# A mixture-of-experts kernel on one core: VectorE's order around the final routing, and who makes the first expert's last low parts

## The reference, cut to what matters

```python
logits = einsum('bsd,de->bse', x, w_gate)
local_gate = sigmoid(x @ w_local)
for s in range(S):
    fresh_e = argmax(logits[b, s])
    e = fresh_e if s == 0 or local_gate[b, s] < 0.5 else prev_e
    prev_e = e
    p = softmax(logits[b, s])
    h = maximum(x[b, s] @ w1[e], 0)
    out[b, s] = p[e] * (h @ w2[e])
```

## Time and profile before

| | |
|---|---|
| median of 3 runs (lowest, highest) | 622.44 us (621.17, 623.4) |
| the profiled execution, its own time | 623.0 us |
| its span, first to last instruction | 621.2 us |
| instructions | 14687 |
| TensorE busy | 607.2 us (98%) |
| VectorE busy | 412.6 us (66%) |
| ScalarE busy | 321.5 us (52%) |
| GpSimd busy | 172.5 us (28%) |
| chain that ended last, by engine | TensorE 90%, VectorE 6%, issue 2%, ScalarE 1%, GpSimd 1% |

### The profile page before, as it was taken

One profiled execution on the slowest core, in us unless ns is written; L12 is line 12 of the kernel. 1 busy time (PEld: TensorE's weight loads), 2 busy tenths in 40 slices (PEclk: granted clock), 3 DMA queues, 4 the chain that ended last, 5 costly groups with the idle time before them and its releaser, 6 DMA issues.

```text
span 621.2 us, 14687 instructions
## 1 busy us (share of the span) xinstructions
PE 607.2 (98%) x4483; PEld 504.5 (81%) x4484; DVE 412.6 (66%) x1164; ACT 321.5 (52%) x698; POOL 172.5 (28%) x241
## 2 busy tenths in 40 slices
PE   7989999999999999999999999999999999999996
PEld 6878888888888888889979878788788888888885
DVE  4767779845888797786979958957735335463541
ACT  5767779768516614632544844637526225362531
POOL 4545545600000000000000231285632521544141
PEclk9999999999999999999999999999999999999999
DMA  8987786002120010000004751886933512754000
GB/s 307 377 272 249 268 288 212 18 2 85 57 80 0 1 51 18 0 34 35 0 21 168 247 227 52 285 305 221 328 127 106 213 62 81 256 197 154 17 17 15
DMA packets 32935, 84.66 MB, mean 136 GB/s; under 512 B 4602, under 2 KB 7418, under 8 KB 32896
## 3 DMA queue, kind: packets, MB, share of 16 engines
q1 hardware_dynamic: 26816, 70.03, 32.5%
q0 software_dynamic: 3200, 8.92, 4.1%
q10 hardware_dynamic: 2880, 5.24, 2.6%
HBM read 76.04 MB, written 9.70 MB: 138 GB/s over the span
## 4 chain that ended last, share of the span: by engine, by line
PE 90%; DVE 6%; issue 2%; ACT 1%; POOL 1%; DVEq 0%; ACTq 0%; POOLq 0%
PE banks L889 23%; PE banks L891 23%; PE banks L890 23%; PE banks L760 3%; PE banks L1079 3%; PE banks L827 2%; DVE we_lo L1531 2%; PE banks L836 2%; PE banks L790 2%; PE banks L774 1%; PE banks L804 1%; PE banks L998 1%; PE banks L800 1%; PE banks L851 1%; DVE neg L1209 1%
## 5 line engine op out<-in xcount | busy, mean ns | idle before, releaser
L1498 DVE CUSTOM_DVE_ANT_0 product<-x,xT 128x512 f32<-128x512 f32 x120 | 77.8, 687 | 1.2 <-DMA xT<-in_w 1.2
L1800 ACT ACTIVATE prob<-neg,negmax 128x160 f32<-128x160 f32 (+1 forms) x136 | 59.1, 436 | 29.7 <-DVE negmax L1209 20.1
L1778 DVE TENSOR_SCALAR hid<-banks 128x512 f32<-128x512 f32 x34 | 23.5, 690 | 72.6 <-PE banks L891 71.5
L889 PE MATMUL banks<-we_hi,hid_hi 128*128 (+1 forms) x160 | 66.4, 415 | 1.6 <-DVE hid_lo L1611 1.6
L1910 ACT ACTIVATE k_sum<-banks 128x512 f32<-128x512 f32 (+2 forms) x40 | 21.4, 534 | 89.4 <-PE banks L891 84.7
L889 PE MATMUL banks<-we_hi,xg_hi 128*128 (+1 forms) x160 | 64.6, 404 | 1.3 <-DVE we_lo L1531 1.3
L891 PE MATMUL banks<-we_hi,xg_lo 128*128 (+1 forms) x160 | 62.6, 391 | 0.0
L891 PE MATMUL banks<-we_hi,hid_lo 128*128 (+1 forms) x160 | 62.6, 391 | 0.0
L890 PE MATMUL banks<-we_lo,hid_hi 128*128 (+1 forms) x160 | 62.6, 391 | 0.0
L890 PE MATMUL banks<-we_lo,xg_hi 128*128 (+1 forms) x160 | 62.4, 390 | 0.0
L686 POOL MEMSET xg<- 128x1024 f32 x1 | 1.0, 956 | 219.3 <-ACT k_raw L1903 219.3
(11 more groups left out here) (295 smaller groups left out, 1465.0 us busy)
## 6 DMA issues: line engine op xcount, KB each, us to landing
xT<-in_w_e SPq DMA_DIRECT2D x36, 512.0 KB, 4.4
raw_end<-in_w_e SPq DMA_DIRECT2D x36, 512.0 KB, 4.9
qk<-in_qk_t SPq DMA_DIRECT2D x32, 448.0 KB, 6.3
vw<-in_v_t SPq DMA_DIRECT2D x32, 256.0 KB, 5.4
w_raw<-in_w_mix ACTq DMA_DIRECT2D x20, 256.0 KB, 4.1
x_rows<-x SPq DMA_DIRECT2D x17, 256.0 KB, 2.0
xT<-in_w SPq DMA_DIRECT2D x8, 256.0 KB, 3.4
vz<-in_v_z SPq DMA_DIRECT2D x8, 128.0 KB, 3.5
```

What stands on the lines that cost most here:

```text
L889: pe.matmul(dst, left[0], right[0], start=first, stop=False)
L1498: dve.tensor_tensor_reduce(product[:, k % 2, :], x2[:, t, :], w9(e), 1.0, 0.0, ALU.mult, ALU.add, dot[:, t % 2, e:e + 1]).then_inc(dotted, 1)
L1778: dve.tensor_scalar(hid[:, D * h:D * (h + 1)], ps_h[:, h, :], 0.0, None, ALU.max).then_inc(hid_ready, 1)
L1800: act.activation(prob[:, t % 2, c], neg[:, c], ACT.Exp, scale=-1.0, bias=negmax[:, t % 2, k:k + 1], accum_out=rsum[:, t % 2, k:k + 1]).the ...
```

## The change

- GpSimd no longer makes the low parts 6 and 7 of the first expert, nor waits for its first six. VectorE makes them, behind the last x2 multiplication; part 5 is now behind it too.
- On VectorE, `choices(final)`, `chosen_left` and `pick` come ahead of the low part of tile 0's second half of hidden, and tile 1's low rows come behind the scan of the counts.
- On TensorE, `turn_chosen` comes one block earlier in tile 0, `count_picks` where it was.
- Part 0 of expert 1 moves on VectorE from ahead of the slot list to behind the gates; there tile 2's low rows follow it, and then parts 1 to 3.
- The gathers of tiles 2 and 3 read their row numbers from `slot_token` itself, without a copy.
- `turn_rows` of tile 2 comes ahead of the last output block of tile 1 on TensorE, and on ScalarE the rounding of those rows ahead of the copy of tile 1's y.

```diff
@@ GpSimd
-            pool.wait_ge(we_lo_ready, VPARTS + VPARTS)
-            last_parts(0, slice(0, 1))
             pool.wait_ge(slots_ready, 2)
             for t in range(GT):
                 pool.wait_ge(x2_stored[t], 16 * sum(t < n for n in SIZES))
+            def first_gather(i, b):
+                pool.sem_inc(rows_in_ready, 1)
+                pool.indirect_dma_start(out=xg[:, b, :], out_offset=None, in_=x2_d[0:TOK, :],
+                                        in_offset=bass.IndirectOffsetOnAxis(ap=slot_token[:, i:i + 1], axis=0),
+                                        bounds_check=TOK - 1, oob_is_err=False).then_inc(gathered[b], 16)
+
             for b in range(EARLY):
                 pool.wait_ge(xg_turned, b + 1)
-                gather(EARLY + b, b, TOK)
+                first_gather(EARLY + b, b)
@@ TensorE
             turn_carries(final)
-            outputs(0, 0, first, range(1, 3))
+            outputs(0, 0, first, range(1, 2))
             turn_chosen(final)
-            outputs(0, 0, first, range(3, 4))
+            outputs(0, 0, first, range(2, 4))
             count_picks(final)
             outputs(0, 0, first, range(4, FC)).then_inc(y_summed, 1)
...
             turn_hidden(1, 1)
-            outputs(1, 0, first, range(1, FC)).then_inc(y_summed, 1)
+            outputs(1, 0, first, range(1, FC - 1))
             turn_rows(2, 0, 1)
+            outputs(1, 0, first, range(FC - 1, FC)).then_inc(y_summed, 1)
             keep_clock(IDLE_TURNS // 4)
@@ VectorE
-            for j in range(PARTS // 2, VPARTS):
+            for j in range(PARTS // 2, VPARTS - 1):
                 rest_of_part(0, slice(0, 1), j)
             last_x2(1)
+            for j in range(VPARTS - 1, PARTS):
+                rest_of_part(0, slice(0, 1), j)
...
             carries(final)
-            rest_of_hidden(0, 1)
             choices(final)
-            rest_of_rows(1)
...
                               ALU.is_equal).then_inc(pick_ready, 1)
+            rest_of_hidden(0, 1)
             own = done(dve.tensor_tensor(work[:], iota_e[:].unsqueeze(1).broadcast_to([P, NT, E]), by_token(chosen, E),
...
             scanned = done(dve.tensor_tensor_scan(flat(upto[:]), flat(first_c[:]), flat(total[:]), 0.0, ALU.mult, ALU.add))
+            rest_of_rows(1)
             after(scanned)
...
             rest_of_hidden(1, 0)
-            dve.wait_ge(x2_turned, 2)
-            for t in range(2):
-                dve.wait_ge(x2_stored[t], 16 * GROUPS)
-            rest_of_part(1, slice(1, 2), 0)
             dve.wait_ge(route_pe, 12)
             slots(slot_of, LATER, slot_token[:, EARLY:MT])
             rest_of_hidden(1, 1)
...
             dve.wait_ge(rows_in_ready, 2 * EARLY)
+            dve.wait_ge(x2_turned, 2)
+            for t in range(2):
+                dve.wait_ge(x2_stored[t], 16 * GROUPS)
+            rest_of_part(1, slice(1, 2), 0)
+            rest_of_rows(2)
             for j in range(1, PARTS // 2):
                 rest_of_part(1, slice(1, 2), j)
-            rest_of_rows(2)
@@ ScalarE
             round_hidden(1, 1)
+            round_rows(2)
             copy_y(1)
-            round_rows(2)
```

## The result

| | before | after |
|---|---|---|
| median of 22 runs each | 622.14 us | 623.8 us |
| ratio, 95% interval | | 1.0037 (1.0026 to 1.0048), +2.3 us (1.6 to 3.0) |
| profiled execution, span | 623.0, 621.2 us | 625.36, 623.5 us |
| TensorE busy | 607.2 us | 610.0 us |
| longest wait of TensorE in the reordered stretch | 1.3 us | 3.2 us |

The account below looks back on a forecast made before the run. TensorE, busy 98%, was taken as the bound, with VectorE's chain paid in full from 384.5 to 409.3 us. A restart +1.65 later, less 0.5 from the earlier x2, gave +1.15, taken as +1.2: 623.6 us median, range 621.3 to 626.0.

Parts of the forecast that it names:

- main case: TensorE restarts on tile 2 later, clock at 1.00, nothing given back: +1.2 us (+0.4 to +2.1); chance 0.50.
- The last x2 ahead of part 5: Near 361 us: TensorE turns the last x2 at 361.3 without a wait, so all that follows starts 0.5 us earlier.
- Low parts from GpSimd to VectorE: First expert's last low parts fit VectorE's 3.69 us of idle time before the logits and cost nothing; otherwise 2.35 us.
- Final choice: Near 370 us: the chosen row is ready before TensorE needs it, so TensorE gains 0.3 us.
- Slot list: On VectorE: complete at 383.25 instead of 383.95, before taking off 0.5; near 382.8 in the changed profile.
- Gather: Tile 2's gather starts 0.9 us earlier without a copy, near 383.7 in the changed profile; its landing shifts alike.
- The bill: TensorE restarts at 392.7, not 391.52: one more part +1.16, new wait with lost overlap +0.8, lead −0.3, earlier x2 −0.5.
- What follows: Behind the restart all work shifts together in unchanged order; nothing is added, and from 409 us nothing gives time back.
- The clock: Rival: the granted clock falls in TensorE's hole of about 3.2 us, costing 2 more: +3.2, 625.6 us; chance 0.28.
- theory A: From the experiments: late low parts and a clock fall in TensorE's rest add up; no keepers +3.2 to +3.8, 33 keepers +0.9.
- Rows, not parts, free TensorE: Rival: TensorE lacked only tile 2's rows at 391.52, so it would start at 389.3: −2.2, 620.2 us; chance 0.07.
- It evens out: Rival: VectorE's lateness is taken up before 409 us: −0.8 to +0.4, near 622.2 us; chance 0.15.

Follow-up runs that it names:

- experiment 3: Before, with only the last x2 ahead of low part 5 and the first expert's last low parts moved from GpSimd to VectorE: 621.71 us, ratio 0.9997.
- experiment 4: After, with expert 1's low part 0 right behind the slot list and part 1 ahead of tile 2's rows on VectorE: 623.27 us, ratio 1.0023.
- experiment 7: Before, with x2 and first-expert low parts as in experiment 3, last x2 behind part 5, expert 1's part 1 made early, first expert-2 load later: 620.91 us.
- Experiment 5: As experiment 4, with SyncE's first load of expert 2 held back until low part 1 is made: 621.53 us, ratio 1.0006 to before.
- experiment 1: After, with 33 instead of 9 clock keepers of TensorE before its wait for expert 1's low parts: 622.33 us, ratio 1.0006 to before.
- 8: After, with expert 1's parts 0 to 3 ahead of tile 2's rows, expert 2's load held until the gather landed, tile 2's relu earlier: 619.72 us.

## Why the prediction was right, and where it was off

**The number.** 623.6 us was forecast, 623.8 measured, in the range of 621.3 to 626.0. That they lie so close is luck in part. What was forecast is +1.2 on a median of 622.44 from three runs; what was measured is +2.3 by the ratio, or +1.7 between the medians, on one of 622.14. And the measured time is the sum of two terms of which my main case had one. The restart alone (+0.95) is less than what was measured, and restart and clock together (+0.95 and 1.6 to 2.8) is somewhat more than the ratio's +2.3, as it would be if the clock fell in most executions and not in all. The change falls just above 0.3%, on the side to which I gave 0.37. Of the signs that I named for being wrong one is there, the granted clock below 1.00 near 392.

**Step by step.**
- *The last x2 ahead of part 5.* Right: turned at 361.26 without a wait (forecast 361.3), 0.5 us gained at the turn, and experiment 3 has it alone (0.6 at the slot matmuls).
- *Low parts from GpSimd to VectorE.* Right: free.
- *Final choice.* Right but for a tenth: turned at 370.42, 0.1 behind TensorE's pace. TensorE's lead at the slot matmuls is 0.85 us, 0.8 forecast.
- *Slot list.* Complete at 382.60, forecast 382.8.
- *Gather.* Started at 383.50, forecast 383.7. The 0.87 us that I kept ahead of an indirect DMA stays after a wait (0.90 here), but between two gathers without a copy it is 0.30. What I had not seen is that a weight load close to the gather can delay its landing: experiment 4 has 4.7 us with a load 0.54 behind it, experiment 7 has 4.6 with two ahead of it, before 3.5 with one 1.7 ahead, after 3.4 with none. The change moves part 0, and with it that load, behind the gather. I shifted the landing by the issue and called ±0.9 its bounds; in after it held.
- *The bill.* VectorE's new wait for the rows is 0.31 us, not 0.7, and the restart +0.95 (37.31 for 36.36), not +1.15: The rows could be taken at 388.19, some 0.3 earlier than in my sum (rounded at 388.96, less the 0.5), which gives the restart; the wait is shorter also because part 0 ended 0.1 later. The term that matters, one low part more in the chain, is right: parts 0 to 3 and the rows take 5.7 us from 386.65 to 392.33. Experiment 5 shows it from the other side: with part 0 back in VectorE's idle time (part 1 ahead of the rows and the load held back) the restart is at 36.36 again.
- *What follows.* Right: from the restart on nothing gives time back or takes more, the last matmul follows at 223.9 ± 0.3.
- *The clock.* This is the step that failed: the main case holds the clock at 1.00 through a hole of 3.2 us and puts its cost at nothing. I gave the fall 0.28 as a rival with the price of 2 us; it came in three profiles of three, at 1.6 to 2.8 us. The row to weigh more was the earlier trace rows, a fall within 2.9 us of rest, against a hole that I had worked out to 3.2; that the clock held in a hole of 1.29 says nothing on 3.2. With the fall taken as the main case the forecast would have been 625.6, over the measured median by 1.8. The timed executions say why in part. Of after's 22, 17 have a mean granted clock of 0.997 or less, with a mean of 624.4 us, and five 0.998 or more, with 623.2. Some 7 us at 1.2 GHz, as in the first profile of after, take 0.005 of a mean over 623 us, and the shorter fall of the third leaves 0.997; a fall elsewhere counts too, as at the end of the span of before (0.998 in its first profile). So the count is rough, but it orders the kernels as theory A does: six of six without keepers, none of 12 with 33, three of 73 of before (those that ran beside the experiments). So the fall was the usual case, not the 0.28 that I gave it. The two groups are 1.2 us apart, but by their scatter it could be 0.2 to 2.2, so that whether a fall costs less there than in the profiles stays open.

**The rivals.** "Rows, not parts, free TensorE" is false for after: its rows are turned at 31.8 and the restart is at 37.3. In experiments 4 and 7, with parts out of the way, the rows' landing did become the bound, in 4 through VectorE's wait for them ahead of its parts 2 and 3. "It evens out" is false: the restart is late, and from there to the last matmul nothing is taken up (223.9 us with the clock held, before and after alike).

As for the sizes: of the ratio's 2.3 us, the reordering itself makes 0.95 by the profiles (experiment 1: 0.4, −0.4 to 1.1, by the runs), and the rest, some 1.4, is the clock that the wider hole cost.

## What to carry to other kernels

When work is moved off an engine's idle time to get a result out sooner, look for what filled that idle time to stand later in the chain; here a low part of 1.16 us was moved out of a free slot into the one stretch where VectorE was the bound. A hole of the matmul engine has a price beyond its length once it is wide enough for the clock, so cost the two apart and test them apart by filling the hole with idle turns. And a step that frees a buffer frees a transfer with it: ask which small, urgent DMA the large one will meet.

## What the runs showed of the hardware that I had not expected

- The length of TensorE's rest alone does not say whether the granted clock falls. It fell around rests of 3.1 to 3.2 us (three of three), 4.2, and once of two at 2.0; in after's last window it still read 1.00 some 4.6 us past the last matmul (618.90 to 623.5), while before's fell within 2.9. The Trainium skill, "TensorE: Matmul & The Clock Gate", section "What's actually happening", says that the low level is the resting state and activity lifts it; the return to 1.00 near 398 under dense matmuls agrees.
- A fall can come after the rest, with TensorE at work again for some 1.5 us (the third profile of after, restart at 392.99; the window 394 to 395 still has 0.76).
- An indirect gather landed 1.3 us later when a 512 KB load went out 0.54 us behind it, on another queue (experiment 4; with the load held back, experiment 5, it didn't).
- The issue of a gather took 1.21 us instead of 1.00 when it began while VectorE made a low part, and ended 0.9 us after that part (experiments 4, 5 and 8).
- An indirect DMA starts 0.90 us after the semaphore that frees it, but 0.30 us behind another one that needs no wait.
